# Input products of two MLPs by one level of Strassen's scheme, behind a long convolution, on one core

## Chip, cores and metric

One core of a Trainium2 chip. The metric is device time in microseconds of one execution, the median of the runs; lower is better.

## What is computed

A circular convolution along the sequence by Fourier transform, and two MLPs of the same size behind it, all in float32:

```python
X = np.fft.rfft(x, axis=1)                       # x: 2 x 3008 x 256
y = np.fft.irfft(X * (filt_r + 1j * filt_i)[None], n=3008, axis=1)
h = y.reshape(6016, 256) @ moe_w_in              # 256 x 2048
y = np.maximum(0.01 * h, h) @ moe_w_out          # 2048 x 256
h = y @ moe2_w_in
out = np.maximum(h, 0.0) ** 2 @ moe2_w_out
```

## The kernel before

The kernel has two stages, written out by hand for each engine, with semaphores between them.

**Transform stage.** The transform of length 3008 = 64 x 47 is done by matmuls. `over_n1` (line 442) transforms over 64; then come 32 units, each with `turn` (line 460, a transpose), `spectrum` (line 471, the forward transform over 47), the product with the filter on VectorE (lines 348, 352, 355), one addition on GpSimd (line 202) and `inverse` (line 483). After unit 16, and again at the end, `turn_back` (line 493) and `sequence` (line 504) bring the result into the tokens' order; ScalarE copies between them (`turned_back`, line 249) and VectorE copies the end result into YT (line 364). SP loads the tables TB and FL of each unit (lines 154, 155) into a ring of FSLOTS = 6 places; a place is free when the unit six back has done its inverse product (`u_ps`). Between them SP loads the first MLP's weights in 16 chunks of 512 columns (line 165). ScalarE rounds each chunk (line 253), and GpSimd takes the rest (line 197).

**MLP stage.** The values are kept channels by tokens: 256 channels are two blocks of 128 partitions, tokens lie along the free axis, 11 tiles of 512 and one of 384. Every product is made of three passes, because an operand is held as a rounded part (H) and a rest (L) in fp32r (lines 552 to 554):

```python
nc.tensor.matmul(acc, wh, xh, start=first, stop=False)
nc.tensor.matmul(acc, wh, xl, start=False, stop=False)
return nc.tensor.matmul(acc, wl, xh, start=False, stop=last)
```

For each tile and each of 16 hidden chunks of 128, `up` makes h from 2 channel blocks (6 matmuls), and `down` adds the chunk's part to the output's 2 blocks (6 matmuls). TensorE's order is fixed: `down` of a chunk, then `up` of the one three ahead (LAG = 3). First MLP: ScalarE makes 0.01 h (line 303), VectorE the maximum (403), the rounding (405) and the rest (412). Second MLP: ScalarE makes relu(h) (305) and its rounded square (307), VectorE the square (410) and the rest (412). Once in a tile, ScalarE copies the outputs of the tile before into YT (line 279) and rounds the next input (line 276), and VectorE takes its rest (line 381). Both MLPs have room for their weights, 64 KB a partition each; the second's come in 16 chunks through one staging place during the first (lines 171, 321, 420). Inner tiles are in a hardware loop, one body for two tiles. Output leaves SP tile by tile (line 174), and the last tile in two halves (lines 177, 179).

Of the kernel before, what the change touches and what calls it, by code (L numbers as in the profile page):

```python
# [26 lines left out]

def fft_mlp_kernel(nc, x, filt, dft, tab, w1, w2, out):
# [11 lines left out]
    o_w1 = 48 * KB  # L40
    o_w2 = o_w1 + 64 * KB
    o_buf = o_w2 + 64 * KB

    X = at("X", [128, B, MH, D], f32, 0)
    UT0 = at("UT0", [128, B, MH, 128], f32, o_w1 + 40 * KB)
    TT1 = at("TT1", [128, 2, B, NJ, K2], f32, o_w2)
    UT1 = at("UT1", [128, B, MH, 128], f32, o_w2)
    V = at("V", [128, 2, 512], f32, o_w2 + 48 * KB)
    STG1 = at("STG1", [128, WSLOTS, W1CH], f32, o_w2 + 52 * KB)
    o_fl = o_buf + FSLOTS * 2 * TBW * 4  # L50
    o_s2 = o_fl + FSLOTS * 4 * 128 * 4
    TB = at("TB", [KR, FSLOTS, 2, TBW], f32, o_buf)
    FL = at("FL", [KR, FSLOTS, 2, 2 * 128], f32, o_fl)
    S2 = at("S2", [K2, 2, B, 2, 128], f32, o_s2)
    YF = at("YF", [KR, 3, B, 2 * 128], f32, 24 * KB)
    XF = at("XF", [KR, 2, B, 2 * 128], f32, 30 * KB)
    DM = at("DM", [128, 3, 128], f32, o_s2 + 4 * KB)

    YT = at("YT", [128, 2, TOK], f32, 0)
    W1H = at("W1H", [128, WCOLS], f32r, o_w1)  # L60
    W1L = at("W1L", [128, WCOLS], f32r, o_w1 + 4 * WCOLS)
    W2H = at("W2H", [128, WCOLS], f32r, o_w2)
    W2L = at("W2L", [128, WCOLS], f32r, o_w2 + 4 * WCOLS)
    YL = at("YL", [128, 2, TOK], f32r, 0)
    XH = at("XH", [128, 2, 2, TILE], f32r, o_buf)
    GH = at("GH", [128, 4, TILE], f32r, o_buf + 16 * TILE)
    GL = at("GL", [128, 4, TILE], f32r, o_buf + 32 * TILE)
    TT = at("TT", [128, 2, TILE], f32, o_buf + 48 * TILE)
    STG2 = at("STG2", [128, WCH], f32, o_buf + 56 * TILE)

    with ExitStack() as ctx:
# [23 lines left out]
        w1_raw = [sem(f"w1_raw{g}") for g in range(WSLOTS)]  # L95
        w1_hi = sem("w1_hi")
        w1_lo = sem("w1_lo")
        w2_raw = sem("w2_raw")
        w2_hi = sem("w2_hi")
        w2_lo = sem("w2_lo")  # L100
        xs_hi = sem("xs_hi")
        xs_lo = sem("xs_lo")
        up_done = sem("up_done")
        t_done = sem("t_done")
        g_done = sem("g_done")
        hi_done = sem("hi_done")
        sq_hi_done = sem("sq_hi_done")
        lo_done = sem("lo_done")
        down_done = sem("down_done")
        evac_done = sem("evac_done")  # L110
        last_half = sem("last_half")
# [11 lines left out]
        W1_LOAD = [0, 1, 2, 3, 4, 5, 7, 9, 11, 13, 17, 18, 19, 20, 21, 22]  # L123
        W1_HI = [3, 4, 5, 6, 7, 8, 10, 12, 13, 15, 20, 21, 22, 23, 24, 25]
        W1_LO = {5: (0,), 7: (1,), 9: (2,), 11: (3,), TURN: range(4, 10), 23: (10,), 25: (11,), 27: (12,), UNITS - 1: (13, 14, 15)}
# [4 lines left out]
        def width(tile):  # L130

            return REST if isinstance(tile, int) and tile % TILES == TILES - 1 else TILE

        def columns(a, tile):

            return a[:, :, bass.ds(tile * TILE, width(tile))]

        @block.sync
        def _(sp):
# [11 lines left out]
            def load_filter(i):  # L151
                if i >= FSLOTS:
                    sp.wait_ge(u_ps, i - FSLOTS + 1)
                sp.dma_start(TB[:, i % FSLOTS, :, :], tab[:, i % PAIRS, :, :]).then_inc(ft_in[i % FSLOTS], 16)
                sp.dma_start(FL[:, i % FSLOTS, :, :], filt[:, i, :, :]).then_inc(ft_in[i % FSLOTS], 16)
# [3 lines left out]
            for i in range(UNITS):  # L159
                load_filter(i)  # L160
                if i - FSLOTS in W1_LOAD:
                    c = W1_LOAD.index(i - FSLOTS)
                    if c >= WSLOTS:
                        sp.wait_ge(w1_lo, c - WSLOTS + 1)
                    sp.dma_start(STG1[:, c % WSLOTS, :], w1[:, c * W1CH:(c + 1) * W1CH]).then_inc(w1_raw[c % WSLOTS], 16)

            sp.wait_ge(up_done, 1)
            sp.dma_start(STG2[:, :], w2[:, 0:WCH]).then_inc(w2_raw, 16)
            with sp.Fori(1, WCOLS // WCH) as c:
                sp.wait_ge(w2_lo, c)  # L170
                sp.dma_start(STG2[:, :], w2[:, bass.ds(c * WCH, WCH)]).then_inc(w2_raw, 16)
            with sp.Fori(0, TILES - 1) as t:
                sp.wait_ge(evac_done, t + (TILES + 1))
                sp.dma_start(out[:, :, bass.ds(t * TILE, TILE)], columns(YT, t)).then_inc(out_done, 16)

            sp.wait_ge(last_evac, 1)
            sp.dma_start(out[:, 0, TOK - REST:], YT[:, 0, TOK - REST:]).then_inc(out_done, 16)
            sp.wait_ge(evac_done, 2 * TILES)
            sp.dma_start(out[:, 1, TOK - REST:], YT[:, 1, TOK - REST:]).then_inc(out_done, 16)
            sp.wait_ge(out_done, 16 * (TILES + 1))  # L180

        @block.gpsimd
        def _(pool):

            nc.gpsimd.memset(X[64:128, :, MH - 1, :], 0.0).then_inc(x_pad, 1)

            pool.wait_ge(x_pad, 1)
            pool.wait_ge(p_ps, 1)
            nc.gpsimd.memset(XF[32:IM, :, :, :], 0.0).then_inc(xf_pad, 1)

            def split_w1(c):

                pool.wait_ge(w1_hi, c + 1)
                if c >= 4:
                    pool.wait_ge(v_ps, c - 3)
                w = slice(c * W1CH, (c + 1) * W1CH)
                nc.gpsimd.tensor_tensor(W1L[:, w], STG1[:, c % WSLOTS, :], W1H[:, w].bitcast(f32), ALU.subtract).then_inc(w1_lo, 1)

            for i in range(UNITS):

                pool.wait_ge(prod, 3 * i + 3)
                nc.gpsimd.tensor_tensor(YF[:, i % 3, :, :], YF[:, i % 3, :, :], XF[:, i % 2, :, :], ALU.add).then_inc(yf_sb, 1)  # L202
                for c in W1_LO.get(i, ()):
                    split_w1(c)

        def n1_out(c, half):

            v = TT1[:, half, c // 6, :, :].rearrange("p j n -> p (j n)").rearrange("p (q m) -> p q m", m=MH)
            return v[:, :, 4 * (c % 6):4 * (c % 6) + 4]


        def pairs(eng, mlp, body):
            first = mlp * TILES // 2
            last = first + TILES // 2 - 1
            body(first)
            with eng.Fori(first + 1, last) as i:
                body(i)
            body(last)

        def piece(i, p, u):  # L220


            k = {(0, 7): 0, (0, 12): 1, (1, 7): 2, (1, 12): 3}.get((p, u))
            if k is None or isinstance(i, int) and i == TILES // 2 - 1 or k == 3 and not isinstance(i, int):
                return None
            return k if isinstance(i, int) else 3 * i + 1 + k

        @block.scalar
        def _(act):
# [21 lines left out]
            def split_w1(c):  # L251
                act.wait_ge(w1_raw[c % WSLOTS], 16 * (c // WSLOTS + 1))
                nc.scalar.activation(W1H[:, c * W1CH:(c + 1) * W1CH], STG1[:, c % WSLOTS, :], ACT.Copy).then_inc(w1_hi, 1)  # L253
# [3 lines left out]
            for i in range(UNITS):  # L257
# [10 lines left out]
                if i in W1_HI:  # L268
                    split_w1(W1_HI.index(i))
# [3 lines left out]

            def split_x(tile, slot):

                nc.scalar.activation(XH[:, slot, :, 0:width(tile)], columns(YT, tile), ACT.Copy).then_inc(xs_hi, 1)

            def evac(tile, slot):
                nc.scalar.activation(columns(YT, tile), PS[:, 4 + 2 * slot:6 + 2 * slot, 0:width(tile)],
                                     ACT.Copy).then_inc(evac_done, 1)  # L280

            for c in range(CH, 2 * CH):
                turned_back(c)
                if c == CH + 3:
                    act.wait_ge(y_sb, CH + 1)
                    split_x(0, 0)
            act.wait_ge(y_sb, 2 * CH)

            def tiles(mlp):
                def body(i):  # L290
                    for p in range(2):
                        t = 2 * i + p
                        first = isinstance(i, int) and t == 0
                        last = isinstance(i, int) and t == 2 * TILES - 1
                        local = t - mlp * TILES
                        for u in range(FCH):
                            s = t * FCH + u
                            h, g = PS[:, u % 4, 0:width(t)], TT[:, u % 2, 0:width(t)]
                            act.wait_ge(up_done, s + 1)
                            if not (isinstance(i, int) and s < 2):  # L300
                                act.wait_ge(lo_done, s - 1)
                            if mlp == 0:
# [427 lines left out]
```

## Time and profile before

| | |
|---|---|
| runs, median of 3 | 1170.44 us (1167.06 to 1172.78) |
| profiled execution: span from first to last instruction | 1166.7 us; its time around the span is not listed |
| matmuls | 5600: 992 in the transform stage, 4608 in the MLP stage |
| first matmul of the MLP stage | starts at 138.54 us |
| busy: TensorE, VectorE, ScalarE, GpSimd | 1153.2, 730.3, 461.3, 62.1 us |
| granted TensorE clock | 1.00 over the span |

PE is TensorE, PEld its weight loads (beside the matmuls), DVE is VectorE, ACT ScalarE, POOL GpSimd, SPq the queue of SP. A digit is the busy share of a fortieth of the span, in tenths. "Idle before" is the time in which an engine waited, with the one that released it behind the arrow.

### The profile page before, as it was taken

Reading aid. Unit: us, or ns where it says so; the run is one execution under the profiler, and the core shown is the slowest. Engines: PE = TensorE matmul, PEld = TensorE weight load, DVE = VectorE, ACT = ScalarE, POOL = GpSimd, SP = SyncE. Lnnn points to the kernel's source line nnn. Section 1 sums busy time; section 2 is a strip of 40 time slices with the busy share of each in tenths; the row PEclk is TensorE's granted clock in tenths of the full one; section 3 lists DMA queues with packets and bytes.
Section 4 is the critical chain, followed back from the end, with each engine's and each line's share of the span. In section 5 each row is a group of like instructions: output and inputs, shape, how many; then the busy total and the mean of one; then the engine's idle time right before and its main releaser. Section 6 shows DMA issues by size and latency. Waiting matters only on the chain.

```text
span 1166.7 us, 15228 instructions
## 1 busy us (share of the span) xinstructions
PE 1153.2 (99%) x5600; PEld 980.0 (84%) x5600; DVE 730.3 (63%) x1133; ACT 461.3 (40%) x757; POOL 62.1 (5%) x54
## 2 busy tenths in 40 slices
PE   7999999999999999999999999999999999999998
PEld 6899988888888888888889888888888888888888
DVE  1879577677677677677667555545545555555554
ACT  2455423233223222222222445545545545545544
POOL 0576100000000000000000000000000000000000
PEclk9999999999999999999999999999999999999999
DMA  9866000000000000000000000000000000000000
GB/s 229 239 171 183 11 10 9 19 16 4 9 18 3 6 18 7 2 18 0 1 1 1 1 1 19 19 1 19 18 0 18 18 0 18 18 0 18 19 1 32
DMA packets 18185, 34.77 MB, mean 30 GB/s; under 512 B 2144, under 2 KB 6112, under 8 KB 18144
## 3 DMA queue, kind: packets, MB, share of 16 engines
q1 hardware_dynamic: 18000, 34.02, 10.6%
q8 instruction: 26, 0.43, 0.2%
q10 hardware_dynamic: 144, 0.20, 0.1%
q14 instruction: 15, 0.12, 0.0%
HBM read 28.05 MB, written 6.16 MB: 29 GB/s over the span
## 4 chain that ended last, share of the span: by engine, by line
PE 96%; DMA 2%; SPq 1%; POOL 0%; issue 0%; ACT 0%; DVE 0%; DVEq 0%
PE PS L552 29%; PE PS L554 29%; PE PS L553 29%; PE PS L471 2%; PE PS L483 2%; PE PS L504 2%; DMA X<-in_x 1%; SPq L147 1%; PE PS L460 1%; PE PS L493 1%; DMA STG<-in_w 0%; PE PS L442 0%; POOL YF L202 0%; DVE XF L355 0%; ACT W1H L253 0%
## 5 line engine op out<-in xcount | busy, mean ns | idle before, releaser
L410 DVE TENSOR_TENSOR TT<-TT 128x512 f32<-128x512 f32 (+1 forms) x192 | 130.8, 681 | 232.2 <-ACT GH L307 232.2
L412 DVE TENSOR_TENSOR GL<-TT,GH 128x512 fp32r<-128x512 f32 (+1 forms) x384 | 261.4, 681 | 13.2
L303 ACT ACTIVATE TT<-PS 128x512 f32<-128x512 f32 (+1 forms) x192 | 113.2, 589 | 368.4 <-PE PS L554 331.3
L403 DVE TENSOR_TENSOR TT<-PS,TT 128x512 f32<-128x512 f32 (+1 forms) x192 | 130.6, 680 | 133.4 <-ACT TT L303 133.4
L305 ACT ACTIVATE TT<-PS 128x512 f32<-128x512 f32 (+1 forms) x192 | 113.2, 589 | 252.7 <-DVE GL L412 154.2
L552 PE MATMUL PS<-GH,W1H 128*128 128x512 f32 (+1 forms) x384 | 147.7, 385 | 0.0
L552 PE MATMUL PS<-XH,W1H 128*128 128x512 f32 (+1 forms) x384 | 147.7, 385 | 0.0
L554 PE MATMUL PS<-XH,W2L 128*128 128x512 f32 (+1 forms) x384 | 147.7, 385 | 0.0
L553 PE MATMUL PS<-YL,W2H 128*128 (+2 forms) x384 | 147.7, 385 | 0.0
L554 PE MATMUL PS<-GH,W1L 128*128 128x512 f32 (+1 forms) x384 | 147.7, 385 | 0.0
L553 PE MATMUL PS<-GL,W1H 128*128 128x512 f32 (+1 forms) x384 | 147.7, 385 | 0.0
L554 PE MATMUL PS<-XH,W1L 128*128 128x512 f32 (+1 forms) x384 | 147.6, 384 | 0.0
L553 PE MATMUL PS<-YL,W1H 128*128 (+2 forms) x384 | 147.6, 384 | 0.0
L552 PE MATMUL PS<-XH,W2H 128*128 128x512 f32 (+1 forms) x384 | 147.6, 384 | 0.0
L554 PE MATMUL PS<-GH,W2L 128*128 128x512 f32 (+1 forms) x382 | 147.0, 385 | 0.0
L553 PE MATMUL PS<-GL,W2H 128*128 128x512 f32 (+1 forms) x382 | 147.0, 385 | 0.0
L552 PE MATMUL PS<-GH,W2H 128*128 128x512 f32 (+1 forms) x382 | 146.9, 385 | 0.0
L307 ACT ACTIVATE GH<-TT 128x512 fp32r<-128x512 f32 (+1 forms) x192 | 119.7, 623 | 6.1
L405 DVE CAST GH<-TT 128x512 fp32r<-128x512 f32 (+1 forms) x192 | 81.1, 422 | 6.5
L552 PEld LDWEIGHTS PS<-GH,W1H 128*128 128x128 f32 x384 | 72.1, 188 | 14.0 <-DVE GL L412 0.4
L553 PEld LDWEIGHTS PS<-YL,W1H 128*128 128x128 f32 x384 | 72.1, 188 | 13.9
L552 PEld LDWEIGHTS PS<-XH,W1H 128*128 128x128 f32 x384 | 72.1, 188 | 13.8
(55 smaller groups left out, 1248.1 us busy)
## 6 DMA issues: line engine op xcount, KB each, us to landing
STG<-in_w SPq DMA_DIRECT2D x32, 256.0 KB, 3.1
FL<-in_filt SPq DMA_DIRECT2D x32, 224.0 KB, 5.1
TB<-in_tab SPq DMA_DIRECT2D x32, 182.0 KB, 3.9
X<-in_x SPq DMA_DIRECT2D x22, 256.0 KB, 8.8
out_y<-YT SPq DMA_DIRECT2D x11, 512.0 KB, 3.1
X<-in_x SPq DMA_DIRECT2D x2, 192.0 KB, 11.3
out_y<-YT SPq DMA_DIRECT2D x2, 192.0 KB, 2.0
DM<-in_dft ACTq DMA_DIRECT2D x1, 192.0 KB, 2.7
```

The costliest lines, as they stand in the source:

```text
L303: nc.scalar.activation(g, h, ACT.Copy, scale=0.01).then_inc(t_done, 1)
L305: nc.scalar.activation(g, h, ACT.Relu).then_inc(t_done, 1)
L307: nc.scalar.activation(GH[:, u % 4, 0:width(t)], g, ACT.Square).then_inc(sq_hi_done, 1)
L403: nc.vector.tensor_tensor(g, PS[:, u % 4, 0:width(t)], g, ALU.max).then_inc(g_done, 1)
L405: nc.vector.tensor_copy(hi, g).then_inc(hi_done, 1)
L410: nc.vector.tensor_tensor(g, g, g, ALU.mult).then_inc(g_done, 1)
L412: nc.vector.tensor_tensor(GL[:, u % 4, 0:width(t)], g, hi.bitcast(f32), ALU.subtract).then_inc(lo_done, 1)
L471: mm = nc.tensor.matmul(PS[0:KR, 2 + i % 2, :].rearrange("p (b k d) -> p b k d", b=B, k=2)[:, :, k, :], TB[0:K2, i % FSLOTS, k, 0:KR], S2[ ...
L483: mm = nc.tensor.matmul(PS[:, 4 + i % 2, col:col + K2], YF[:, i % 3, b, 128 * k:128 * k + 128], TB[:, i % FSLOTS, k, KR:], start=True, sto ...
L552: nc.tensor.matmul(acc, wh, xh, start=first, stop=False)
L553: nc.tensor.matmul(acc, wh, xl, start=False, stop=False)
L554: return nc.tensor.matmul(acc, wl, xh, start=False, stop=last)
```

## The change

**Input products.** Two hidden chunks and two token tiles are taken together: a 2 x 2 block product, done by Winograd's form of Strassen's scheme with 7 products in place of 8. Both MLPs have NP = 6 pairs of tiles (widths 512, 512, 480, twice) and KU = 8 pairs of hidden chunks: 8 slots a pair of tiles, SLOTS = 96. With B for input blocks and A for weight blocks, S and T for their sums, the four h blocks C are built in PSUM and by VectorE:

```diff
+    def wi_forms(mlp, k):                                    # GpSimd
+        nc.gpsimd.tensor_tensor(f[4], f[3], f[2], ALU.add).then_inc(wi_s, 1)
+        nc.gpsimd.tensor_tensor(f[5], f[4], f[0], ALU.subtract).then_inc(wi_s, 1)
+        nc.gpsimd.tensor_tensor(f[6], f[1], f[5], ALU.subtract).then_inc(wi_s, 1)
+        nc.gpsimd.tensor_tensor(f[3], f[0], f[3], ALU.subtract).then_inc(wi_s, 1)
...
+    def x_forms(p):                                          # GpSimd, four of 512
+        ...
+            pool.wait_ge(p3_ps, (p - 1) * KU)
+        nc.gpsimd.tensor_tensor(t1, b12, b11, ALU.subtract).then_inc(xf_t, 1)
+        nc.gpsimd.tensor_tensor(b12, b22, b12, ALU.subtract).then_inc(xf_t, 1)
+        nc.gpsimd.tensor_tensor(t2, b22, t1, ALU.subtract).then_inc(xf_t, 1)
+        nc.gpsimd.tensor_tensor(t4, b21, t2, ALU.subtract).then_inc(xf_t, 1)
...
+    XB = (2, 3)
+    YB, ZB = 0, 1
+    group_a(s): wait h_sb[UD] s-1; P1 -> XB[s % 2]; wait h_sb[UA] s;  P2 -> YB
+    group_b(s): wait s1_sb s+1;   P6 += XB;         wait h_sb[UC] s;  P7 -> ZB
+    group_c(s): wait s2u_sb s+1;  P5 += XB
+    group_d(s): wait s7_sb s+1, h_sb[UB] s+1;       P4 += ZB;         P3 += XB
...
+    for s in range(SLOTS - 1):                               # TensorE
+        group_a(s)
+        down(4 * s - LAG)
+        if s >= 1:
+            group_d(s - 1)
+        down(4 * s - LAG + 1)
+        group_b(s)
+        down(4 * s - LAG + 2)
+        group_c(s)
+        down(4 * s - LAG + 3)
```

(The four `group_` lines are written shorter than in the code; each product has three passes.) `down` keeps its 6 matmuls a block, four blocks (units A, B, C, D) a slot, LAG = 6 units behind. In the last slot the order is A, D of the slot before, down, B, down, C, down, D, then seven downs.

**Elementwise work of a slot.** ScalarE keeps snapshots of P1, P1 + P6 and P7 in SN (`snap1`, `snap2`, `snap7`) and copies C12 (`whole_d`). VectorE adds: C11 = P2 + SN0 (`whole_a`), C22 = XB + SN2 (`whole_b`), C21 = ZB + SN1 (`whole_c`). All land in a ring GF of six places, which a unit may enter when the `down` six units back is done. VectorE makes the activation in place in one scalar_tensor_tensor, ScalarE rounds it to GH, VectorE takes the rest to GL:

```diff
+    for s in range(SLOTS + 1):                               # VectorE
+        if s >= 1:
+            g_act(s - 1, UB)
+            g_split(s - 1, UB)
+        if s < SLOTS:
+            whole_a(s)
+            g_act(s, UA)
+        if s >= 1:
+            whole_c(s - 1)
+        if s < SLOTS:
+            g_split(s, UA)
+        if s >= 1:
+            g_act(s - 1, UD)
+            g_act(s - 1, UC)
+            g_split(s - 1, UD)
+            g_split(s - 1, UC)
+        if s < SLOTS:
+            whole_b(s)
...
+    # ScalarE's order: snap1(s), round B(s-1), [evacuate t1], round A(s), whole_d(s-1), [evacuate t2],
+    # snap2(s), round D(s-1), snap7(s), round C(s-1), [wo_round] [wi_round] [x_round]
```

**Inputs and weights.** GpSimd makes the forms of inputs and weights and their rests (`x_split`, `wi_split`, `wo_split`), but for the first pair, where VectorE takes YL in two pieces behind its last `sequence`. ScalarE rounds (`x_round` in four pieces, `wi_round` 7 x 128 wide, `wo_round` 512 wide). Input weights of the first MLP come during the transform (8 loads in place of 16); three chunks are formed at unit 16, the other five in the first slots. All output weights are loaded when the last `sequence` is done. The second MLP has no room of its own: each of its chunks goes to the first MLP's place:

```diff
+    for k in range(KU + 1):                                  # SP
+        if k < KU:
+            sp.wait_ge(p3_ps, last1 + k + 1)
+            sp.dma_start(WIF[:, k, 0:4, :], w2i[:, k, :, :]).then_inc(wi_raw[k], 16)
+        if k >= 1:
+            sp.wait_ge(down_ps, unit(last1 + k - 1, UD) + 1)
+            sp.dma_start(WOF[:, k - 1, :], w2o[:, k - 1, :]).then_inc(wo_raw[k - 1], 16)
...
+    if KU * (NP - 1) + 6 <= s < KU * (NP - 1) + 6 + KU:      # ScalarE, at the end of its slot
+        wi_round(1, s - KU * (NP - 1) - 6)
+    if KU * (NP - 1) + 7 <= s < KU * (NP - 1) + 7 + KU:
+        wo_round(1, s - KU * (NP - 1) - 7)
```

**Also.** FSLOTS goes from 6 to 5. GpSimd's weight work at unit 16 stands ahead of its addition for unit 17. ScalarE's rounding for the first pair stands behind each of its last four `turned_back`. The hardware loops are gone; all slots are written out. Outputs leave in pieces of two tiles.

## Rows read from the trace of the kernel before

**Rows 1.** Page: busy time, share, instructions; then busy tenths by fortieth of the span
```profile
PE 1153.2 (99%) x5600; PEld 980.0 (84%) x5600; DVE 730.3 (63%) x1133; ACT 461.3 (40%) x757; POOL 62.1 (5%) x54
...
POOL 0576100000000000000000000000000000000000
PEclk9999999999999999999999999999999999999999
```
**Rows 2.** Page: chain that ended last, by engine, then by line
```profile
PE 96%; DMA 2%; SPq 1%; POOL 0%; issue 0%; ACT 0%; DVE 0%; DVEq 0%
```
**Rows 3.** Waits over the span: waiting, releaser, us in total, times, longest
```profile
PEld PS L552 <- DVE GL L412: 0.4, 1, 0.4
```
**Rows 4.** Groups by form, TensorE: count, busy us, mean ns, idle before
```profile
L552 PE MATMUL PS<-GH,W1H 128*128 128x512 f32 x352 | 137.0, 389 | 0.0
```
**Rows 5.** Timeline of TensorE, inner tile and last tile: start us, duration us
```profile
600.18 0.39 PE L553 MATMUL PS<-GL,W1H 128*128 128x512 f32 x1
600.41 0.39 PE L554 MATMUL PS<-GH,W1L 128*128 128x512 f32 x1
...
1161.13 0.33 PE L552 MATMUL PS<-GH,W2H 128*128 128x384 f32 x1
1161.30 0.33 PE L553 MATMUL PS<-GL,W2H 128*128 128x384 f32 x1
```
**Rows 6.** Timeline at the handover: ScalarE copies, last VectorE copy, first MLP product
```profile
132.82 0.60 ACT L249 ACTIVATE V<-PS 128x512 f32<-128x512 f32 x1 [0.73 <-PE PS L493]
...
136.81 0.60 ACT L249 ACTIVATE V<-PS 128x512 f32<-128x512 f32 x1 [0.73 <-PE PS L493]
...
138.54 0.47 PE L552 MATMUL PS<-XH,W1H 128*128 128x512 f32 x1
```
**Rows 7.** Timeline at the end: last product, last copy, last output issue
```profile
1163.03 0.34 PE L586 MATMUL PS<-GL,W2H 128*128 128x384 f32 x1
...
1164.23 0.43 SPq L179 DMA_DIRECT2D out_y<-YT  x1
```
**Rows 8.** Groups by form, elementwise: count, busy us, mean ns, idle before
```profile
L410 DVE TENSOR_TENSOR TT<-TT 128x512 f32<-128x512 f32 x176 | 121.9, 693 | 216.8 <-ACT GH L307 216.8
...
L307 ACT ACTIVATE GH<-TT 128x512 fp32r<-128x512 f32 x176 | 111.3, 632 | 5.6
...
L352 DVE SCALAR_TENSOR_TENSOR XF<-PS,FL 48x512 f32<-48x512 f32 x32 | 22.2, 693 | 1.3 <-POOL XF L189 0.3
...
L197 POOL TENSOR_TENSOR W1L<-STG,W1H 128x512 fp32r<-128x512 f32 x16 | 20.3, 1274 | 2.4 <-PE PS L493 2.1
L381 DVE TENSOR_TENSOR YL<-YT,XH 128x1024 f32 x16 | 19.5, 1219 | 0.0
...
L276 ACT ACTIVATE XH<-YT 128x1024 fp32r x16 | 16.8, 1050 | 0.0
```
**Rows 9.** Timeline: a filter load's issue, and the spectrum product at the fourth unit behind
```profile
90.42 0.31 SPq L154 DMA_DIRECT2D TB<-in_tab  x1
...
95.01 1.03 PE L471 MATMUL PS<-S,TB 96*112 96x256 f32 x4
```
**Rows 10.** DMA issues from 74 to 80 us and from 103 to 109: median us to landing
```profile
FL<-in_filt SPq DMA_DIRECT2D x2, 224.0 KB, 3.1
...
FL<-in_filt SPq DMA_DIRECT2D x3, 224.0 KB, 6.0
```
**Rows 11.** Timeline: GpSimd's splits at the turn, the next inverse product, GpSimd's last work
```profile
75.86 7.90 POOL L197 TENSOR_TENSOR W1L<-STG,W1H 128x512 fp32r<-128x512 f32 x6 [2.12 <-PE PS L493]
...
89.36 1.03 PE L483 MATMUL PS<-TB,YF 112*128 112x96 f32 x8
...
119.59 3.73 POOL L197 TENSOR_TENSOR W1L<-STG,W1H 128x512 fp32r<-128x512 f32 x3
```
**Rows 12.** Timeline of VectorE: its first operation with two SBUF inputs
```profile
131.59 1.22 DVE L381 TENSOR_TENSOR YL<-YT,XH 128x1024 fp32r<-128x1024 f32 x1
```
**Rows 13.** Timeline of TensorE while the input arrives: idle time before in brackets
```profile
27.40 1.16 PE L442 MATMUL PS<-DM,X 128*128 128x128 f32 x8 [1.03 <-DMA X<-in_x]
```

More of the change, by code:

```diff
@@ L128, in fft_mlp_kernel, with pair_cols, width, cols @@
         UT = [UT0, UT1]
[L130 to L136, printed above, removed]
+        def pair_cols(p):
+            q = p % NP
+            b, i = q // len(PAIR_W), q % len(PAIR_W)
+            return b * S + 2 * sum(PAIR_W[:i]), PAIR_W[i]
+        def width(s):
+            return PAIR_W[s // KU % len(PAIR_W)]
+        def cols(a, d, t, p):
+            c, w = pair_cols(p)
+            return a[:, d, c + t * w:c + t * w + w]
+        def unit(s, kind):
+            return 4 * s + kind
+        UA, UB, UC, UD = range(4)
         @block.sync
@@ L160, in _ @@
                 load_filter(i)
[L161 to L171, printed above, removed]
@@ L172, in _ @@
-            with sp.Fori(0, TILES - 1) as t:
-                sp.wait_ge(evac_done, t + (TILES + 1))
-                sp.dma_start(out[:, :, bass.ds(t * TILE, TILE)], columns(YT, t)).then_inc(out_done, 16)
+                if i - FSLOTS in WI_LOAD:
+                    k = WI_LOAD[i - FSLOTS]
+                    sp.dma_start(WIF[:, k, 0:4, :], w1i[:, k, :, :]).then_inc(wi_raw[k], 16)
+            sp.wait_ge(y_ps, 2 * CH)
+            for k in range(KU):
+                sp.dma_start(WOF[:, k, :], w1o[:, k, :]).then_inc(wo_raw[k], 16)
@@ L202, in _, with g_slot @@
                 nc.gpsimd.tensor_tensor(YF[:, i % 3, :, :], YF[:, i % 3, :, :], XF[:, i % 2, :, :], ALU.add).then_inc(yf_sb, 1)
-                for c in W1_LO.get(i, ()):
-                    split_w1(c)
+                if i == TURN:
+                    for k in range(3):
+                        wi_forms(0, k)
+                    for k in range(3):
+                        wi_split(0, k)
+            x_forms(0)
+            x_split(0)
+            for k in range(KU):
+                wo_split(0, k)
+                if k + 3 < KU:
+                    wi_forms(0, k + 3)
+                    wi_split(0, k + 3)
+                if k == 1:
+                    x_forms(1)
+                if k == 5:
+                    x_split(1)
+            for p in range(2, NP + 1):
+                x_forms(p)
+                x_split(p)
+            for k in range(KU + 1):
+                if k < KU:
+                    wi_forms(1, k)
+                    wi_split(1, k)
+                if k >= 1:
+                    wo_split(1, k - 1)
+                if k == 3:
+                    x_forms(NP + 1)
+                if k == 7:
+                    x_split(NP + 1)
+            for p in range(NP + 2, 2 * NP):
+                x_forms(p)
+                x_split(p)
         def n1_out(c, half):
-            v = TT1[:, half, c // 6, :, :].rearrange("p j n -> p (j n)").rearrange("p (q m) -> p q m", m=MH)
+            v = TT1[half][:, c // 6, :, :].rearrange("p j n -> p (j n)").rearrange("p (q m) -> p q m", m=MH)
             return v[:, :, 4 * (c % 6):4 * (c % 6) + 4]
[L212 to L226, printed above, removed]
+        XB = (2, 3)
+        YB, ZB = 0, 1
+        def g_slot(n):
+            return n % RING
         @block.scalar
@@ L272, in _ @@
                         turned_back(c)
[L274 to L280, printed above, removed]
+                        if c in (5, 6, 7):
+                            wi_round(0, c - 5)
             for c in range(CH, 2 * CH):
@@ L424, in _, with whole_a @@
[L424 to L428 removed]
+            x_split(1)
+            x_split(0)
+            def whole_a(s):
+                n, w = unit(s, UA), width(s)
+                dve.wait_ge(p2_ps, s + 1)
+                dve.wait_ge(s1_sb, s + 1)
+                if n >= RING:
+                    dve.wait_ge(down_ps, n - RING + 1)
+                nc.vector.tensor_tensor(GF[:, g_slot(n), 0:w], PS[:, YB, 0:w], SN[:, 0, 0:w], ALU.add).then_inc(h_sb[UA], 1)
@@ L625, in _, with up @@
-            tiles(0)
-            tiles(1)
+            def up(s, bank, form, hi, lo, first):
+                k, x, w = s % KU, s // KU % 2, width(s)
+                acc, wh, wl, xh = PS[:, bank, 0:w], WIH[:, k, form, :], WIL[:, k, form, :], XH[x][:, hi, 0:w]
+                nc.tensor.matmul(acc, wh, xh, start=first, stop=False, skip_group_check=not first)
+                nc.tensor.matmul(acc, wh, lo, start=False, stop=False, skip_group_check=not first)
+                return nc.tensor.matmul(acc, wl, xh, start=False, stop=True, skip_group_check=not first)
@@ L629, in dft_tables @@
+            group_c(s)
+            down(4 * s - LAG + 2)
+            group_d(s)
+            for n in range(4 * s - LAG + 3, 4 * SLOTS):
+                down(n)
 def dft_tables():
```

532 lines of the change are left out of this document (313 added, 219 removed).

## Prediction

> **What bounds the kernel now.** I first read busy time by engine [rows 1]: TensorE works 1153 of 1166.7 us, VectorE 63% and ScalarE 40% of the span, GpSimd 5%. In the slices TensorE is at 9 or more nearly everywhere with its clock at full, 2.4 GHz, throughout, while the GpSimd digits are zero after the first 11%. The chain of work that ended last [rows 2] says that this occupation is also the limit: 96% of it is TensorE and 88% the three lines of the MLP products (552, 553, 554). In the MLP stage the list of waits [rows 3] has engines waiting for TensorE and for each other, but TensorE waits once, 0.4 us. So a matmul removed there is worth its whole slot, as long as the others keep ahead.
>
> What a matmul is worth must come from start to start: the 389 ns of a 512-column matmul [rows 4] overlaps the next one. In the timeline [rows 5] starts are 0.227 us apart at 512 columns and 0.173 at 384. Check: 4224 x 0.2266 + 384 x 0.1735 = 1023.8 us, and the stage runs from 138.54 [rows 6] to 1163.2 us [rows 7], 1024.6. Straight lines between the two give 0.2133 us at 480 columns.
>
> **TensorE's work.** Before, two hidden chunks by two token tiles cost 24 + 24 matmuls (up, down). After, the seven products of the scheme cost 7 x 3 = 21, the outputs still 24: 45 a slot. 96 slots make 4320 matmuls, 2880 at 512 and 1440 at 480 columns: 2880 x 0.2266 + 1440 x 0.2133 = 959.8 us. Gain 64.0 us (3/48 of the stage). A full slot takes 10.20 us at 512.
>
> **Does the rest of a slot fit under 10.20 us?** VectorE: three recombinations, four activations, four splits: 11 operations. Its nearest rows are 0.69 us whatever the operand's place [rows 8], 0.725 with the gap; the activation as scalar_tensor_tensor with both inputs in SBUF isn't shown, but the same operation from PSUM takes 693 ns and the tensor_tensor with two SBUF inputs 693, so I take that: 8.0 us. The cast falls away. ScalarE: three snapshots and one copy out of PSUM at 0.60, four roundings at 0.63: 4.9 us, plus 1.05 for an evacuation of 1024 columns or 1.05 + 0.95 + 0.63 for the rounding of input, input weights and output weights: under 7.6 us [rows 6, 8]. GpSimd: 1.27 us per 512 elements, so for each pair four forms 5.1 us and splits of 3584 elements 8.9 us, 14 us in 80; in the weight slots another 1.6 + 2.2 + 1.3 = 5.1 us of 10.2 (the four 128-wide forms aren't shown; I take 0.4 us each, between a quarter of 1.27 and 1.27 itself). Throughput fits everywhere.
>
> Then latency, by laying the order out by hand from these rows, slot start = 0. The first product is free for ScalarE at 0.9. VectorE's whole_a must wait for the output product that frees its ring place, done at 2.72 + 0.25, so 2.97 to 3.70; activation to 4.42; whole_c to 5.15. TensorE wants that at 6.12, where P7 overwrites the single Z bank: 0.9 us to spare. P5 wants the second snapshot (6.97) at 8.16: 1.2 to spare. P4 wants whole_b of the slot before, done at 0.2, at 2.72. The split of unit C ends at 9.7, wanted 1.36 us into the slot after. The evacuation waits at the second slot of each pair stand before the snapshot and leave 0.8. So, if operations last as in these rows, the steady slots cost nothing beyond TensorE: 0 us, bounds 0 and 0.3 us a slot (29 us).
>
> **The transform stage.** The ring of filter tables has five places, not six. A load is issued when the inverse product five units back ends, and its spectrum product comes two turns and 0.44 us later, 4.8 us; before it had 7.0. An issue at 90.42 [rows 9] would be needed at 95.01. Filter loads land after 3.1 us with a quiet queue and 6.0 with weight loads between [rows 10]; these loads fall from 16 to 8, so I expect some 3.5 us, and the table's issue stands ahead: it just fits. I take 1 us, bounds 0 and 1.2 us on 27 units (32). At the turn, ScalarE's three wide roundings push the transposes by 0.5 us, and GpSimd's three weight splits now end near 89.2 where six narrower ones end at 83.7 [rows 11], with the YF addition for the inverse product at 89.36 queued behind them: 1.2 us. That weight loads no longer hold up ScalarE is credited with nothing. Sum +2.7 us.
>
> **Handover.** Today the last transform product runs straight into the first MLP product [rows 6]. Now ScalarE rounds four pieces between its last four copies. From the copy at 132.8, each of 0.60 with 1.05 behind it, the last copy ends at 138.35 instead of 137.41 and the last product 0.85 us later, copied by 140.0. Behind it on VectorE stand two splits of 1.22 us [rows 8]: first MLP product at 142.4 instead of 138.54, +3.9. GpSimd's splits end at 141.5, inside. SP issues the output weights at about 139.5; they land within the 6 us of [rows 10], before ScalarE comes to them at 147.3.
>
> **First two slots.** Nothing is in flight to cover the chains. P5 waits 1.4 us for the second snapshot, which stands behind the rounding of unit A. Then ScalarE does three output roundings and waits for GpSimd (output split 1.27, forms 1.6) before its input rounding (0.95), with the next first snapshot queued behind: P6 waits 2.35 us. P7 then waits 2.9 us for VectorE's chain split, whole_a, activation, whole_c. With 0.24 at the first P6: 6.9 us, where before 0.3: +6.6, bounds +3 and +12.
>
> **Between the MLPs.** Weights replace their predecessors chunk by chunk: the load waits for the last use in slot 40 + k, forms and rounding come in slot 46 + k, need in slot 48 + k, 2 slots later against 5.1 us of GpSimd work: 0 us. The former copies on ScalarE and VectorE were hidden too.
>
> **End.** In the last slot group D comes before the output product that frees whole_a's place, so whole_a starts at 4.1, and P7 waits 1.8 us; then group D waits 0.85 for whole_b. The tail behind the last product (3.5 us, [rows 7]) stays: +2.7.
>
> **Sum** against the profiled span: 1166.7 - 64.0 + 2.7 + 3.9 + 6.6 + 2.7 = 1118.6. The median of the runs, 1170.4, lies 3.8 above the span (no other time of the profiled execution is listed); 1122.4, so 1122.
>
> **Port rival (slower).** In the rows GpSimd never works while VectorE runs an operation with two SBUF inputs: its work ends at 123.3 [rows 11], the first such operation starts at 131.59 [rows 12], and later it has none [rows 1]. In the transform stage both work side by side at 0.69 and 1.27 us, but there VectorE has one input in PSUM. The change puts 230 us of GpSimd work beside eight such operations a slot. If each blocks the other for its length: the four forms come at 4.4 us into a slot, alternate with VectorE's operations and push the split of unit C 1.5 us past its need; the three 2.5 us splits of a pair start at the end of a slot and delay whole_c, so P7, by 0.6, 1.1 and 1.1 us. That is 5 us a pair, 52 for ten pairs, and some 2.5 us in each of 13 slots with weight work, 32: 1206. Half as much gives 1164. It decides from about 0.9 us of blocking in one slot. Against it speaks only that no row shows any slowing. The Trainium skill, page "SBUF — State Buffer", section "Who interferes with whom", says that a VectorE instruction with two SBUF inputs contends with a GpSimd instruction that reads SBUF, the later one blocked whole, and one with a single SBUF input not; the trace agrees with the second half and cannot show the first. By that rule the sum would be 1206, by the rows as they stand 1122.
>
> **Chain rival (still faster).** The 0.9 us before P7 is spent by hand-offs that I set at 0.06 us between VectorE and ScalarE and 0.25 from TensorE. If whole_c comes 0.3 us late in each slot: 96 x 0.3 = 29 us, 1151.
>
> **Transform rival.** Filter loads land late by 1 us in each unit, or TensorE's clock drops to 1.2 GHz after the 3.9 us of handover and the early waits (full clock after idle times of 1 us, [rows 13]; nothing longer is shown) and doubles the first 5 us of products: 1125 to 1155, still faster.
>
> **How the numbers follow.** Forecast 0.50, port rival 0.30 (0.20 of it slower, 0.05 same, 0.05 faster), chain rival 0.12, transform rival 0.03, anything else 0.05 (0.04 slower). About 0.5% is what a measurement of this kernel can tell from no change, 1164.6 to 1176.3. Faster 0.70 (0.50 + 0.12 + 0.03 + 0.05), same 0.06, slower 0.24. The forecast's own range is 1112 to 1136 from its bounds; to leave out no more than 2 in 10 the range must take in the lower half of the port rival: 1110 to 1182. That the scheme isn't what runs is excluded by 45 matmuls in place of 48.
>
> **What would show it.** Right: 5312 matmuls (4320 + 992), starts 0.227 us apart through the stage, first MLP product near 142.4, TensorE waits that sum to under 15 us and lie in the first two slots and the last, VectorE near 80% and its GF and GL operations at 0.69 us while GpSimd works. Port: the same operations longer or started late whenever GpSimd is busy, GpSimd operations over 1.3 us, TensorE waiting for whole_c or g_lo in the third to sixth slots of each pair and in the weight slots, but not elsewhere. Chain: a wait before P7 in all slots alike. Transform: spectrum products waiting for TB or FL. I am wrong if TensorE waits over 0.2 us in steady slots without GpSimd work, or if its starts are further apart than 0.23 us with nothing waited for.

## The result, and the profile after

The changed kernel takes 1153.59 us (median, 1151.56 to 1154.81), the kernel before 1171.61 us beside it: ratio 0.9852, 95% interval 0.9829 to 0.9874. It is faster by 1.5%, where 4.1% was forecast (1122 for 1170.4). The span of the profiled execution is 1153.0 us, the forecast's own sum 1118.6, so 34 us have to be found.

The page of the changed kernel, busy time and slices, beside [rows 1]:

```profile
PE 1110.2 (96%) x5312; PEld 935.5 (81%) x5312; DVE 898.8 (78%) x1191; ACT 556.5 (48%) x973; POOL 317.2 (28%) x228
...
PE   6999969999999999999999998999999999999997
...
POOL 0356457622022122201213587211211220210000
PEclk9899989999999999999999999899999999999999
```

TensorE has its 5312 matmuls, but is busy for 96% instead of 99%. The missing tenths stand in slice 6 (144 to 173 us) and slice 25 (692 to 721 us), where GpSimd has digits of 5 and more; the clock digit falls in slice 6 and in slice 26, right behind (and in slice 2, while the input arrives). GpSimd is busy five times as long as before. The waits of TensorE and its weight loads show on whom (columns: total, times, longest, in us); before, there was one of 0.4 [rows 3]:

```profile
PEld PS L753 <- DVE GF L583: 13.9, 12, 4.0
PEld PS L745 <- DVE GL L598: 13.8, 13, 5.8
PE PS L753 <- DVE GF L583: 9.9, 6, 3.5
...
PE PS L745 <- DVE GL L598: 8.8, 8, 5.4
```

The windows of the changed kernel tell which stretches lose (after the window: PE, PEld, DVE, ACT, POOL busy us, granted clock, DMA share, GB/s):

```profile
147.00:150.00 3.00, 2.70 (x6) 2.12 (x7) 0.24 (x1) 0.60 (x1) 0.00 (x0) 0.55 0.98 328
...
158.00:169.00 11.00, 6.38 (x18) 4.82 (x19) 8.06 (x10) 6.13 (x11) 7.45 (x7) 0.69 0.00 0
169.00:260.00 91.00, 86.66 (x379) 70.15 (x378) 76.49 (x91) 46.01 (x79) 50.03 (x34) 1.00 0.00 1
260.00:640.00 380.00, 379.19 (x1695) 317.24 (x1694) 311.81 (x416) 189.96 (x333) 73.26 (x46) 1.00 0.03 10
...
716.00:726.00 10.00, 4.62 (x14) 3.34 (x13) 8.86 (x8) 3.38 (x6) 5.61 (x3) 0.74 0.00 1
...
745.00:1120.00 375.00, 374.47 (x1673) 313.02 (x1672) 297.57 (x411) 183.97 (x324) 51.41 (x28) 1.00 0.04 15
```

In the 755 us of the two long windows TensorE idles 1.3 us: the steady slots do nearly what was forecast. The loss sits where weights are formed as well as inputs: the first slots, up to 222 us, and 660 to 730 us, the second MLP's weights.

The cause shows in VectorE's operations. GL is the split, GF<-GF the activation (590 in the first MLP, 592 in the second). Groups by form (busy us, mean ns, idle before):

```profile
L598 DVE TENSOR_TENSOR GL<-GF,GH 128x512 fp32r<-128x512 f32 x256 | 200.0, 784 | 110.2 <-ACT GH L442 101.7
L592 DVE SCALAR_TENSOR_TENSOR GF<-GF 128x512 f32<-128x512 f32 x128 | 122.2, 975 | 2.4 <-ACT GF L436 0.2
L590 DVE SCALAR_TENSOR_TENSOR GF<-GF 128x512 f32<-128x512 f32 x128 | 120.7, 963 | 2.2
```

The same kernel's operations by source line (least, median and longest duration): the in-place activation (592, two SBUF inputs) and `whole_c` (583, one input in PSUM):

```profile
L592 DVE SCALAR_TENSOR_TENSOR GF<-GF x192: 649/685/2878, 644.8 to 1142.1; 128x512 f32<-128x512 f32 x128, 128x480 f32<-128x480 f32 x64
...
L583 DVE TENSOR_TENSOR GF<-PS,SN x96: 645/682/686, 162.8 to 1139.8; 128x512 f32<-128x512 f32 x64, 128x480 f32<-128x480 f32 x32
```

The operation that reads PSUM is never over 686 ns. The activation, with both inputs in SBUF, has the same median, 0.685 us, but single ones last up to 2.88 us; these stand beside GpSimd's splits. The worst stretch, on GpSimd's timeline and on VectorE's (start, duration, us):

```profile
705.71 2.59 POOL L244 TENSOR_TENSOR WIL<-WIF,WIH 128x896 fp32r<-128x896 f32 x1 [2.79 <-ACT WIH L364]
708.26 1.74 POOL L249 TENSOR_TENSOR WOL<-WOF,WOH 128x512 fp32r<-128x512 f32 x1
709.96 5.66 POOL L280 TENSOR_TENSOR YL<-YT,XH 128x1024 fp32r<-128x1024 f32 x2
715.58 4.49 POOL L286 TENSOR_TENSOR XL<-XT,XH 128x1024 fp32r<-128x1024 f32 x2
```

```profile
711.25 2.12 DVE L598 TENSOR_TENSOR GL<-GF,GH 128x512 fp32r<-128x512 f32 x1
713.29 5.65 DVE L592 SCALAR_TENSOR_TENSOR GF<-GF 128x512 f32<-128x512 f32 x2
718.86 3.42 DVE L598 TENSOR_TENSOR GL<-GF,GH 128x512 fp32r<-128x512 f32 x2
```

GpSimd reads without a pause for over 14 us, and its YL splits last 2.83 us each there, for 2.4 at their shortest; two activations need 5.65 us instead of 1.3. TensorE waits for the split behind them, and the clock is down when it goes on: products of 0.80 and 0.63 us for 0.39, and the next start 0.60 us later where 0.23 is usual.

```profile
716.57 0.39 PE L755 MATMUL PS<-XH,WIL 128*128 128x512 f32 x1
722.34 0.80 PE L745 MATMUL PS<-GH,WOH 128*128 128x512 f32 x1 [5.38 <-DVE GL L598]
722.94 0.63 PE L746 MATMUL PS<-GL,WOH 128*128 128x512 f32 x1
```

### The profile page after: what moved, and what is told of

It is laid out like the page before. It is cut to its first block, busy times and chain, and to the rows that moved or that the text cites. A ratio compares the mean times of both kernels' runs of the same rounds, so it can differ in the third digit from the quotient of the medians.

```text
span 1153.0 us, 14228 instructions
## 1 busy us (share of the span) xinstructions
PE 1110.2 (96%) x5312; PEld 935.5 (81%) x5312; DVE 898.8 (78%) x1191; ACT 556.5 (48%) x973; POOL 317.2 (28%) x228
## 4 chain that ended last, share of the span: by engine, by line
PE 78%; DVE 9%; ACT 4%; POOL 3%; issue 3%; DMA 1%; SPq 1%; DVEq 0%
PE PS L745 13%; PE PS L746 12%; PE PS L747 12%; PE PS L753 11%; PE PS L755 11%; PE PS L754 11%; DVE GL L598 2%; PE PS L676 2%; PE PS L664 2%; DVE GF L590 2%; DVE GF L592 2%; ACT GH L442 2%; DMA X<-in_x 1%; PE PS L697 1%; PE PS L653 1%
## 5 line engine op out<-in xcount | busy, mean ns | idle before, releaser
L598 DVE TENSOR_TENSOR GL<-GF,GH 128x512 fp32r<-128x512 f32 (+1 forms) x384 | 287.9, 752 | 165.2 <-ACT GH L442 152.2
L442 ACT ACTIVATE GH<-GF 128x512 fp32r<-128x512 f32 (+1 forms) x384 | 238.5, 621 | 297.6 <-DVE GF L592 149.4
L745 PE MATMUL PS<-GH,WOH 128*128 128x512 f32 (+1 forms) x768 | 298.7, 389 | 8.8 <-DVE GL L598 8.8
L746 PE MATMUL PS<-GL,WOH 128*128 128x512 f32 (+1 forms) x768 | 297.6, 387 | 0.0
L747 PE MATMUL PS<-GH,WOL 128*128 128x512 f32 (+1 forms) x768 | 297.2, 387 | 0.0
L753 PE MATMUL PS<-XH,WIH 128*128 128x512 f32 (+1 forms) x672 | 262.3, 390 | 17.6 <-DVE GF L583 9.9
L755 PE MATMUL PS<-XH,WIL 128*128 128x512 f32 (+1 forms) x672 | 260.3, 387 | 0.0
L590 DVE SCALAR_TENSOR_TENSOR GF<-GF 128x512 f32<-128x512 f32 (+1 forms) x192 | 179.5, 955 | 3.3
L745 PEld LDWEIGHTS PS<-GH,WOH 128*128 128x128 f32 x768 | 144.8, 189 | 41.4 <-DVE GL L598 13.8
L592 DVE SCALAR_TENSOR_TENSOR GF<-GF 128x512 f32<-128x512 f32 (+1 forms) x192 | 171.4, 913 | 4.7 <-ACT GF L436 1.3
L754 PE MATMUL PS<-YL,WIH 128*128 128x512 f32 (+1 forms) x384 | 149.0, 388 | 0.0
```

The source lines that it names most:

```text
L442: nc.scalar.activation(GH[:, g, 0:width(s)], GF[:, g, 0:width(s)], ACT.Copy).then_inc(g_hi[kind], 1)
L590: nc.vector.scalar_tensor_tensor(h, h, 0.01, h, ALU.mult, ALU.max).then_inc(g_sb[kind], 1)
L592: nc.vector.scalar_tensor_tensor(h, h, 0.0, h, ALU.max, ALU.mult).then_inc(g_sb[kind], 1)
L598: nc.vector.tensor_tensor(GL[:, g, 0:w], GF[:, g, 0:w], GH[:, g, 0:w].bitcast(f32), ALU.subtract).then_inc(g_lo[kind], 1)
L753: nc.tensor.matmul(acc, wh, xh, start=first, stop=False, skip_group_check=not first)
L754: nc.tensor.matmul(acc, wh, lo, start=False, stop=False, skip_group_check=not first)
```

## Experiments

All times below are spans of profiled executions unless called a median. The input arrives up to 3 us earlier or later from one execution to the next (TensorE's third wait for it ends at 27.1 us in one profile and 28.8 in another), so the MLP stage is compared by its own length, from the start of its first to that of its last product: 1000.9 us in the changed kernel. These lengths come from one profile each; experiment 5, which leaves the stage as it is, has 1001.5, so a difference under 1 us says nothing. By their ratios to the kernel before, experiments 4 to 8 can't safely be told from the changed kernel: each interval overlaps with its 0.9829 to 0.9874.

**1. Take the reads away.** Each tensor_tensor of GpSimd in the MLP work is replaced by constants written to the same place (the MLPs' values are then wrong), so:

```diff
+            def fill(dst, sem, n):                # n writes, about as long as the read was
...
-                nc.gpsimd.tensor_tensor(WIL[:, k, :, :], WIF[:, k, :, :], WIH[:, k, :, :].bitcast(f32), ALU.subtract).then_inc(wi_lo, 1)
+                fill(WIL[:, k, :, :].bitcast(f32), wi_lo, 3)
```

> The changed kernel, but every GpSimd operation on inputs and weights of the MLPs writes a constant to the same place instead of reading two tensors (the values of the MLPs are then not the reference's), two or three writes for each so that GpSimd stays busy about as long and everything waits for the same things. Port theory (a VectorE operation with two SBUF inputs and a GpSimd operation that reads SBUF exclude each other): VectorE's in-place activations fall from a mean of 963 and 975 ns to 0.69 us and none is over 0.72, the 5.4 us wait of TensorE near 717 us and the clock drop behind it vanish, the two YL operations at the handover take 1.22 us each instead of 1.29 and 2.28; 12 to 17 us come off, a span of 1136 to 1141. Rival (the chains are simply too long where GpSimd's results are awaited, whatever it reads): the waits stay where they are, the span stays within 4 us of 1153.

Measured: span 1127.1 us, median 1131.85, ratio to the kernel before 0.9671 (0.9641 to 0.9700). VectorE, groups by form:

```profile
L606 DVE TENSOR_TENSOR GL<-GF,GH 128x512 fp32r<-128x512 f32 x256 | 177.3, 693 | 167.3 <-ACT GH L450 161.0
L598 DVE SCALAR_TENSOR_TENSOR GF<-GF 128x512 f32<-128x512 f32 x128 | 85.5, 689 | 2.2
```

the activation by source line, with its range:

```profile
L600 DVE SCALAR_TENSOR_TENSOR GF<-GF x192: 649/685/694, 632.2 to 1116.2; 128x512 f32<-128x512 f32 x128, 128x480 f32<-128x480 f32 x64
```

and its window from 660 to 730 us:

```profile
660.00:730.00 70.00, 70.00 (x311) 57.96 (x310) 50.10 (x76) 39.15 (x68) 32.10 (x64) 1.00 0.03 12
```

No activation is over 0.694 us, TensorE has no wait there (61.96 of 70 us busy in the changed kernel), and the MLP stage takes 976.6 us, 24.3 less. GpSimd's own time there is shorter too (32.1 against 49.7 us). The reads of that stretch, each at the shortest that it has in this trace, would take some 39 us (an estimate), so the writes were about a sixth short, and the 24 us are the price of the reads with all that follows from them, not of the lock alone. The direction is that of the port theory and the size is above it (12 to 17 us); the rival, by which the waits stay, is out: from 660 to 730 us there is none.

One part stays. Up to 168 us TensorE still loses 9.0 us without a single read, against 11.4 in the changed kernel; from 168 to 730 us it loses nothing.

**2. Even widths.**

```diff
-PAIR_W = (512, 512, 480)
+PAIR_W = (504, 504, 496)
```

> The changed kernel with tile widths 504, 504, 496 in place of 512, 512, 480 (the same sum). In the changed kernel starts are 0.2270 us apart at 512 columns and 0.2170 at 480, where a straight line from 512 and 384 gave 0.2133. If 480 is a bad width by itself, the new widths lie on the line (0.2234 and 0.2200) and the stage loses up to 5 us. Rival (any width below 512 costs a fixed few ns more in this kernel than on the line): spacings 0.227 and 0.224, and the span grows by about 5 us. If the cost is per matmul and falls on none of the two, it is within 1 us of 1153.

Measured: span 1159.5 us, ratio 0.9913 (0.9884 to 0.9941), MLP stage 8.0 us longer. Mean spacings, waits left out: 0.2275 us at 504 and 0.2234 at 496. The rival is right: 480 isn't a bad width by itself, 496 and 504 lie above the line too. Of the gap between forecast and result, 7 us are spacing: 1440 x (0.2171 - 0.2133) and 2880 x (0.2271 - 0.2266).

**3. The eighth product back.**

```diff
+                up(s, YB, 1, 2, cols(YL, 1, 0, p), True)
                 up(s, YB, 1, 2, cols(YL, 1, 0, p), True).then_inc(p2_ps, 1)
```

> The changed kernel with product P2 made twice (the second overwrites the first), so that a slot has 48 matmuls as before the change; nothing else differs. If the seventh-for-eighth product is worth its whole matmul time (288 matmuls, 64 us) in this kernel, the span is about 1153 + 64 - what the longer slot takes off the waits at the two bursts (up to 8): 1209 to 1217, above the kernel before. Rival (the saving is eaten by VectorE, which then has the slack back): 1165 to 1185.

Measured: span 1202.2 us, ratio 1.0285 (1.0250 to 1.0320), 49.2 us over the changed kernel: outside both forecasts, and nearer the first. The 288 matmuls cost 64.4 us at their spacing; the time that TensorE loses by waits and low clock in the stage falls from 34.4 to 19.9 us. So the scheme's whole saving is there, and 14.5 us of it were given back to waits, because 10.2 us are less room for the rest of a slot than 10.9. The same run says that the kernel would have lost without the scheme: with as many matmuls as before, everything else that the change brings costs about 33 us (ratio 1.0285).

**4. Spread the burst.** In `x_split` the pieces are taken singly: `if 4 <= k <= 7: x_split(NP + 1, (k - 4,))` instead of all at k = 7.

> The changed kernel, but the four GpSimd input splits for the second pair of the second MLP, which stand together behind the last input-weight split, are taken one by one behind the weight splits of chunks 4 to 7, when each is ready. Theory (the 5.4 us wait near 717 us is a burst: seven long GpSimd reads in a row lock VectorE's activations out; with slack between they are absorbed): the wait goes, with the half clock behind it, and little comes up at chunks 4 to 7: 5 to 8 us less, a span of 1145 to 1148. Rival (the locked time is the same wherever it stands): the wait is spread over four slots, the span stays within 2 us of 1153.

Measured: span 1151.0 us, median 1152.81, ratio 0.9843 (0.9816 to 0.9869), MLP stage 0.9 us shorter. The window:

```profile
660.00:730.00 70.00, 63.03 (x261) 49.25 (x260) 59.48 (x64) 35.42 (x61) 50.01 (x35) 0.98 0.00 1
```

The 5.4 us wait is gone, but TensorE is busy for 63.0 us instead of 62.0: waits of 1.1, 1.1 and 2.1 us take its place, and the clock still falls behind the last of them, for half as long. The rival is right. A slot with 5 us of weight reads has no room for another 2.5 wherever they stand.

**5. The turn.**

```diff
-                    for k in range(3):
-                        wi_split(0, k)
+                    wi_split(0, 0)
+                if i in (TURN + 2, TURN + 4):
+                    wi_split(0, (i - TURN) // 2)
```

> The changed kernel, but of GpSimd's three input-weight splits at unit 16 two are moved behind the additions of units 18 and 20, so that the addition of unit 17 no longer stands behind all three. Theory: the 1.8 us that TensorE waits near 93.5 us is this order; it goes, the transform stage and the span get 1.8 to 2.2 us shorter, nothing else moves. Rival (the wait moves to the units where the splits now stand, 2.1 us each on an engine with 0.9 us free in a unit): no gain, or up to 1 us more.

Measured: span 1147.7 us, median 1149.76, ratio 0.9827 (0.9803 to 0.9852). In the changed kernel and here:

```profile
93.51 1.13 PE L676 MATMUL PS<-TB,YF 112*128 112x96 f32 x8 [1.80 <-POOL YF L292]
```

```profile
96.83 1.13 PE L677 MATMUL PS<-TB,YF 112*128 112x96 f32 x8 [0.40 <-POOL YF L292]
```

The wait shrinks from 1.8 us to 0.4, and moves from the inverse product of unit 17 to that of unit 21, behind a split that was moved. From the first spectrum product to the last `sequence` product it takes 105.1 us instead of 107.5. The rest of the difference in span is the input's arrival.

**6. Two chunks early.** Chunks 3 and 4 are formed and split ahead of `x_forms(0)`; ScalarE rounds them behind the copies CH + 1 and CH + 3.

```diff
+            for k in (3, 4):
+                wi_forms(0, k)
+                wi_split(0, k)
             x_forms(0)
```

> The changed kernel, but chunks 3 and 4 of the first MLP's input weights are formed, rounded and split while GpSimd idles between its last addition and the input forms (124 to 131 us), not in the first two slots. Theory for the start: of 11.4 us that TensorE loses between 147 and 168 us, the 2.5 us wait for the first snapshot of slot 1 (ScalarE stands behind GpSimd's forms) and most of the 3.5 us wait for whole_c with the half clock behind it come from this weight work; 5 to 8 us less, and of the 5.1 us lost from 186 to 222 some 1 to 3 us, since locked-out activations are caught up earlier; the last transform products may come 0.3 us later: a span of 1143 to 1147. Rival (an empty pipeline costs the same whatever else is done): at most 2 us less.

Measured: span 1146.7 us, ratio 0.9807 (0.9781 to 0.9833), MLP stage 994.9 us, 6.1 shorter. Waits of TensorE from 147 to 170 us, changed kernel first:

```profile
PE PS L753 <- DVE GF L583: 3.5, 1, 3.5
PE PS L753 <- ACT SN L414: 2.5, 1, 2.5
```

```profile
PE PS L758 <- DVE GF L588: 2.5, 1, 2.5
PE PS L750 <- DVE GL L603: 1.3, 1, 1.3
```

The snapshot's wait goes, as expected; that for `whole_c` shrinks by 1.0 us only (experiment 1, without reads, still has 2.2 there), and a wait of 1.3 us for a split is new. The transform stage gets 1.1 us longer, where 0.3 was expected: at 132.7 us TensorE waits 1.7 us for one of ScalarE's copies, which have the two roundings between them.

**7. Output-weight splits on VectorE.** `wo_split(1, k)` leaves GpSimd; VectorE does it ahead of `whole_b` in slots 48 to 55.

```diff
+                    dve.wait_ge(wo_hi, KU + k + 1)
+                    nc.vector.tensor_tensor(WOL[:, k, :], WOF[:, k, :], WOH[:, k, :].bitcast(f32), ALU.subtract).then_inc(wo_lo, 1)
```

> The changed kernel, but the eight output-weight splits of the second MLP are done by VectorE (one operation of some 0.7 us in each of slots 48 to 55) instead of by GpSimd (1.7 us each). Port theory: each takes 1.3 to 1.7 us of lock away and gives 0.65 us of work, so the stretch from 660 to 730 us, where TensorE loses 11.5 us, gets 4 to 8 us shorter: a span of 1145 to 1149. Rival (VectorE's own work is what is too long there, 12 operations in a slot of 10.2 us): the same or longer, 1153 to 1158.

Measured: span 1147.9 us, median 1151.59, ratio 0.9844 (0.9820 to 0.9869). The MLP stage is 2.3 us shorter, half of the least I expected. Twelve VectorE operations in a slot cost less than eleven and a GpSimd read; the sign is the port theory's.

**8. The handover.** ScalarE rounds the upper block behind copy 2 CH - 6, the others one copy earlier; VectorE takes the upper rest behind `sequence(2 * CH - 5)`.

> The changed kernel, but for the first pair ScalarE rounds the upper channel block two copies earlier (it doesn't depend on the forms), VectorE takes its rest between two copies, and the other three roundings come one copy earlier. Theory: the first MLP product at 147.3 us waits for two VectorE splits (1.29 and 2.28 us, the second locked out by GpSimd's split) behind the last copy; with one gone and the last copy some 0.5 us earlier the product starts near 145, and with an idle time of about 2 us before it the clock may stay at full, which saves 1.6 us more: 2 to 4.5 us less, a span of 1148.5 to 1151. Rival (GpSimd's splits of the other forms are the last to end): under 1 us.

Measured: span 1148.5 us, median 1150.16, ratio 0.9831 (0.9805 to 0.9856). First MLP product in the changed kernel and here:

```profile
147.30 0.80 PE L753 MATMUL PS<-XH,WIH 128*128 128x512 f32 x1 [4.13 <-DVE YL L549]
147.89 0.63 PE L754 MATMUL PS<-YL,WIH 128*128 128x512 f32 x1
```

```profile
144.22 0.50 PE L759 MATMUL PS<-XH,WIH 128*128 128x512 f32 x1 [2.03 <-DVE YL L554]
144.55 0.40 PE L760 MATMUL PS<-YL,WIH 128*128 128x512 f32 x1
```

The wait falls from 4.1 to 2.0 us and the clock stays up: next start after 0.33 us instead of 0.59. MLP stage 1.4 us shorter for the clock.

**9. All of it.** Edits 4 to 8 together.

> The changed kernel with the edits of e4 to e8 together: GpSimd's weight splits at the turn spread, chunks 3 and 4 formed early, the handover's rounding earlier, output-weight splits of the second MLP on VectorE and the second pair's input splits one by one. If the gains of the single edits add up (MLP stage 1000.9 us: less 6.1, 2.3 and 1.4, and 0 to 3 for the spread splits now that a slot has room; transform and handover less 2 and 2), the span is 1135 to 1142 and beats both kernels by 1% and 2.6%. Rival (the lock only moves, and each edit hands the wait on): above 1145.

Measured: span 1139.1 us, median 1141.93 (1140.88 to 1143.99), ratio 0.9762 (0.9741 to 0.9784) to the kernel before, which has a median of 1169.43 here. It beats both: the changed kernel's ratio was 0.9852 (0.9829 to 0.9874), so it gains another 1%. MLP stage 991.1 us, 9.8 shorter, which is the sum of experiments 6, 7 and 8 (6.1, 2.3, 1.4).

**10. Four widths.** `PAIR_W = (448, 384, 352, 320)`.

> A look at the cost of a matmul by its width: the changed kernel with four pair widths 448, 384, 352 and 320 (the same sum of columns, 128 slots instead of 96, so the time itself tells nothing of the change). Taking columns / 2.4 from the spacing, 512 and 384 columns leave 13.7 and 13.3 ns, 480, 496 and 504 leave 17.1, 16.7 and 17.5. If what counts is a width that is a multiple of 128, 384 leaves 13.5 and 448, 352 and 320 leave 17; if a multiple of 64 is enough, 448 and 320 leave 13.5 too and 352 leaves 17.

Measured, in one profile, at full clock and with waits left out: spacing less columns / 2.4 is 17.7 ns at 448, 13.7 at 384, 14.0 at 352 and 13.3 at 320. Neither rule holds. With the other runs: 13.3 to 14.0 ns at 512 and at 384 and less, 16.7 to 17.7 at 448, 480, 496 and 504. What makes the difference stays open; measured is that the 1440 matmuls of 480 columns cost 5.5 us more than by the line.

## Why the prediction failed in size

**Direction and gain: right.** Faster, and the term of 64.0 us for TensorE's work is there (experiment 3: 64.4). The time lies in the range, and 32 us above the number: the saving is half eaten. (By spans it is 34: I added 3.8 us from span to median, and the listed runs have 1.8.)

**"So, if operations last as in these rows, the steady slots cost nothing".** Nearly right: 1.3 us idle in 755, some 4 us by the distance between starts. The chain rival, 0.3 us in each slot (22 us there), is wrong.

**The step that failed** is what stands behind that "if". I priced VectorE's operations with two SBUF inputs from rows in which GpSimd stands still, and put 0 us between the MLPs and 6.6 into the first slots. The port rival named the mechanism, but I gave it 0.30 and counted nothing of it into the sum. Measured, as time lost by TensorE against its usual spacing: 11.4 us to 168 us and 5.1 more to 222, for a forecast of 6.6; 11.5 us from 660 to 730, for a forecast of 0. By experiment 1 the reads cost 24.3 us of the stage, nearly all of what waits and clock took beyond the forecast.

The rule of the Trainium skill (page "SBUF — State Buffer", section "Who interferes with whom") is that a VectorE instruction with two SBUF inputs contends with a GpSimd instruction that reads SBUF, and not with one that only writes. This trace agrees in both halves: activations with two SBUF inputs up to 2.88 us beside GpSimd's reads, 0.694 beside its writes, recombinations with one PSUM input at most 0.694 throughout.

**A second term, put at nothing: the clock.** The waits of the first slots up to 168 us are 1.0, 2.5 and 3.5 us, 7.0 together, for 6.9 forecast; that this fits so well is partly luck, since without reads they are 5.0 (experiment 1). Most of what lies above is the half clock behind the handover and behind the third wait, which the sum left out and only the transform rival named; experiment 1 has it too.

**The port rival's own price was wrong the other way.** It put 52 us on the input work of ten ordinary pairs (its own parts, 1.5, 0.6, 1.1 and 1.1, make 4.3 us a pair and not 5); the steady windows show some 0.5 us a pair. With its 32 us for weight slots it counted 84; experiment 1 shows 24. The reason is, as far as a steady slot shows, that I stacked durations. ScalarE's timeline in a steady slot of the changed kernel:

```profile
304.12 0.60 ACT L421 ACTIVATE SN<-PS 128x512 f32<-128x512 f32 x1 [0.73 <-PE PS L755]
304.61 0.62 ACT L442 ACTIVATE GH<-GF 128x512 fp32r<-128x512 f32 x1
305.13 0.59 ACT L428 ACTIVATE SN<-PS 128x512 f32<-128x512 f32 x1
305.61 0.63 ACT L442 ACTIVATE GH<-GF 128x512 fp32r<-128x512 f32 x1
```

Operations that don't wait for each other start 0.50 us apart, not 0.62. So ScalarE finishes early, the next split of GpSimd starts 0.8 us before the slot does (at 286.81 for a slot at 287.6) and is over when VectorE comes to its critical operations:

```profile
286.81 2.25 POOL L286 TENSOR_TENSOR XL<-XT,XH 128x960 fp32r<-128x960 f32 x1 [7.93 <-ACT XH L380]
287.20 2.42 DVE L590 SCALAR_TENSOR_TENSOR GF<-GF 128x512 f32<-128x512 f32 x1
```

VectorE idles 1.4 to 1.7 us for unit B's rounding in a slot without reads, and the lock falls mostly into that. In weight slots 5 us of reads come on top. Those alone still fit (TensorE doesn't wait between 680.6 us and the 5.4 us before 722.3); with input work beside them, so that GpSimd reads for some 14 us with hardly a pause, they don't.

**Spacing.** 0.2133 us for 480 columns, by the straight line: 0.2171, with 512 columns 7 us in all. My own sign (starts more than 0.23 us apart with nothing waited for) could not have shown it, since it was set for 512 columns.

**Transform stage and handover.** First product at 147.3 us for 145.1 in the sum (the 142.4 among the signs leaves out the transform's 2.7). The ring of five places costs nothing: the delay against the kernel before falls from 3.0 us to 2.2 over the first 16 units, and TensorE has no wait for TB or FL. The turn costs 2.0 us (forecast 1.7). The handover's wait is 4.1 us, of which 1.1 is lockout (experiment 1: 3.0). About 3 us were the input's later arrival in this execution and the low clock behind it (granted 0.57 from 27 to 35 us), in no term of mine. **End:** waits 2.0 us for 2.65. From the start of the last product to the end it takes 4.7 us for 3.6: the last issue comes 1.5 us behind that start for 1.2, and what follows it takes 3.2 us for 2.4. Why is not shown.

Sum: 7 spacing + 25 waits and clock + 2 up to the first product + 1 at the end = 35, for 34 measured.

## To carry to other kernels

A row's duration holds for the neighbours that it had. Before work goes to GpSimd beside VectorE, ask which VectorE operations read two SBUF tensors, and whether each slot has idle time for the longest GpSimd read: ordinary slots swallowed 2.5 us reads, and slots with 5 us of weight reads did too; with 2.5 us of input reads on top the bounding engine, TensorE, stalled. When a bound is laid out from rows, stack start-to-start distances, not durations, and read the matmul's spacing at the width that will be used.

## What the runs showed of the hardware that was not expected

- GpSimd's reads stretch too: the 512-column input forms take 1.27 us beside VectorE's PSUM copies and 1.42 to 1.67 on the average over the stage.
- TensorE's clock: after idle times of 4.1, 3.5 and 5.4 us it goes on at half (granted 0.55 from 147 to 150 us). After shorter ones it can go either way: no drop after 2.0 us (experiment 8), and none after 3.0 us at 145.8 us in experiment 1; but half clock after 2.2 us at 158.8 us in the same run (1.8 us of idle time shortly before), and from 716.7 us on, behind 2.1 us, in experiment 4. The three drops in the changed kernel's MLP stage cost 1.7, 2.1 and 2.8 us beyond the waits.
- Matmuls of 448 to 504 columns cost 3 to 4 ns more than their columns and a 512-column matmul's overhead; those of 320 to 384 don't; cause open.
